# Attention and two Strassen-like MLPs on one core: order of the reciprocals, of the loads and of one product, and the place of some tiles

## What is computed

```python
scores = cap * np.tanh(scale * (q @ k.T) / cap)
attn = np.exp(scores - max);  attn = attn / (attn.sum(-1) + 1e-9);  x = attn @ v
h = x @ w_in;  g = np.maximum(0.01 * h, h);  x = g @ w_out            # 768 -> 2048 -> 768
xn = x / rms * rms_g;  g = xn @ w_gate;  silu = g / (1 + np.exp(-g))
out = (silu * (xn @ w_val)) @ w_out2                                   # 768 -> 1536 -> 768
```

## Time and profile before

| | us |
|---|---|
| three executions, median | 560.29 |
| lowest, highest | 560.08, 561.92 |
| the profiled execution: device time | 560.67 |
| its span, first to last instruction | 558.9 |
| PE busy | 553.1 (99%) |
| DVE busy | 429.7 (77%) |
| POOL busy | 323.6 (58%) |
| ACT busy | 290.0 (52%) |

### The profile page before, as it was taken

How to read it: one execution, slowest core, us unless ns; L and a number is a source line. 1 busy time by engine, 2 the same in 40 slices (tenths; PEclk the granted TensorE clock), 3 DMA queues, 4 the chain that set the end, 5 groups by cost and what they waited for, 6 DMA issues and landing times.

```text
span 558.9 us, 7933 instructions
## 1 busy us (share of the span) xinstructions
PE 553.1 (99%) x2679; PEld 466.1 (83%) x2679; DVE 429.7 (77%) x594; ACT 290.0 (52%) x503; POOL 323.6 (58%) x282
## 2 busy tenths in 40 slices
PE   8999999999999999999999999999999999999997
PEld 5545554699999999999999999999999999999896
DVE  4459988695677799932159498999999999999963
ACT  6888889326445497431155355444434446824330
POOL 1025365478666653594383576766776896634672
PEclk9999999999999999999999999999999999999999
DMA  6254442123111112213022011122211111210521
GB/s 174 70 177 149 135 133 52 37 72 110 62 56 57 57 57 66 86 38 114 1 62 90 0 58 56 58 65 86 77 56 57 57 57 57 62 52 1 154 91 67
DMA packets 30007, 41.49 MB, mean 74 GB/s; under 512 B 17040, under 2 KB 19088, under 8 KB 29968
## 3 DMA queue, kind: packets, MB, share of 16 engines
q1 hardware_dynamic: 29824, 40.99, 23.7%
q10 hardware_dynamic: 144, 0.00, 0.0%
HBM read 38.15 MB, written 2.80 MB: 73 GB/s over the span
## 4 chain that ended last, share of the span: by engine, by line
PE 90%; DVE 6%; issue 2%; DMA 1%; ACT 0%; DVEq 0%; ACTq 0%
PE ps L1763 46%; PE ps L1848 13%; PE ps L1696 9%; PE ps L1933 8%; PE ps L1835 7%; PE ps L1684 3%; PE ps L1702 2%; PE ps L1688 1%; DVE act_lo L1502 1%; DVE x_lo L1502 1%; DMA qk_raw<-in_qk 1%; DVE x_lo_f L1476 1%; DVE act_full L1482 0%; DMA sums<-x_raw 0%; DVE x_raw L1069 0%
## 5 line engine op out<-in xcount | busy, mean ns | idle before, releaser
L644 POOL TENSOR_TENSOR w_lo<-w_raw,w_hi 128x384 fp32r<-128x384 f32 x109 | 128.6, 1189 | 82.3 <-ACT w_hi L757 81.6
L644 POOL TENSOR_TENSOR w_lo<-s_sum,w_hi 128x384 fp32r<-128x384 f32 x112 | 129.6, 1172 | 78.9 <-ACT w_hi L757 78.8
L1763 PE MATMUL ps<-x_hi,w_hi 128*128 128x448 f32 x420 | 154.1, 367 | 0.0
L1763 PE MATMUL ps<-x_hi,w_lo 128*128 128x448 f32 x420 | 153.5, 365 | 0.0
L1763 PE MATMUL ps<-x_lo,w_hi 128*128 128x448 f32 x420 | 153.4, 365 | 0.0
L757 ACT ACTIVATE w_hi<-s_sum 128x384 fp32r<-128x384 f32 x112 | 57.1, 523 | 125.4 <-DVE s_sum L1132 50.1
L1763 PEld LDWEIGHTS ps<-x_hi,w_hi 128*128 128x128 f32 x420 | 78.9, 188 | 7.3 <-issue 0.7
L1763 PEld LDWEIGHTS ps<-x_hi,w_lo 128*128 128x128 f32 x420 | 78.9, 188 | 6.4
L1763 PEld LDWEIGHTS ps<-x_lo,w_hi 128*128 128x128 f32 x420 | 78.9, 188 | 6.2
L757 ACT ACTIVATE w_hi<-w_raw 128x384 fp32r<-128x384 f32 x109 | 55.0, 512 | 20.2 <-PE ps L1835 10.0
L1696 PE MATMUL ps<-probs,v_ones 128*65 128x448 f32 x144 | 56.6, 540 | 0.3 <-DVE x_raw L1069 0.2
(11 more groups left out here) (220 smaller groups left out, 1086.1 us busy)
## 6 DMA issues: line engine op xcount, KB each, us to landing
w_raw<-in_w_out SPq DMA_DIRECT2D x27, 384.0 KB, 3.5
w_raw<-in_w_in SPq DMA_DIRECT2D x16, 384.0 KB, 3.8
qk_raw<-in_qk SPq DMA_DIRECT2D x11, 480.0 KB, 4.5
w_raw<-in_w_gate SPq DMA_DIRECT2D x12, 384.0 KB, 3.0
w_raw<-in_w_val SPq DMA_DIRECT2D x12, 384.0 KB, 3.7
v_ones<-in_v SPq DMA_DIRECT2D x12, 224.0 KB, 3.2
recip_row<-recips SPq DMA_DIRECT2D x12, 224.0 KB, 3.4
out<-sq SPq DMA_DIRECT2D x6, 224.0 KB, 2.0
```

The source lines that it names most:

```text
L644: pool.tensor_tensor(w_lo[:, c], source, w_hi[:, c].bitcast(F32), ALU.subtract).then_inc(w_lo_done, 1)
L1763: last = pe.matmul(ps[:, base(s) + BANK_OF[j], 0:S], w[:, w_c], x[:, xs(j, c)], start=(j in (P1, P5, P7, P6) and c == 0 and w is w_hi and ...
```

## The change

It has seven parts. (1) In DVE's loop of the pairs, `normalise(p - 2)` stands ahead of `reciprocal(p - 1)`. (2) On SP, q and k of pair 4 are loaded ahead of the loop and those of pair p + 5 behind `store_recip(p)`. (3) On SP, panel p instead of p - 1 is loaded in turn p, and behind `load_recip_row(p)`, for p from 0 to 3. (4) The eight small tiles are laid behind G and `spare`, which moves RING, G and `spare` down by 352 bytes, to multiples of 256 bytes from the base. (5) The low part of (1, `T2`, 2) gets a place of its own, `z_spare` in `spare`; it is made before `z_sum(1, T4, 2)` and waits for it no more. (6) At the joint PE makes `P1` of unit 1 before column 2 of `P3`, `P7` and `P6` of unit 0. (7) The order of counts `pe_order` follows (6).

```diff
-    pe_order = [widx(0, j) for j in (P1, P5, P3, P7)] + [widx(1, P1), widx(0, P6)] + [widx(1, j) for j in (P5, P7, P6)]
+    pe_order = [widx(0, P1), widx(0, P5), widx(1, P1)] + [widx(0, j) for j in (P3, P7, P6)] + [widx(1, j) for j in (P5, P7, P6)]
...
+        RING = place["at"]
+        h_sums = buf("h_sums", 8 * S, F32)
+        G = place["at"]
+        g = buf("g", 2 * N1 * S, F32)
+        SPARE = place["at"]
+        spare = buf("spare", S, F32)
+
         ones = buf("ones", 2, F32)
...
         rms = buf("rms", 3 * 8, F32)
-        RING = place["at"]
-        h_sums = buf("h_sums", 8 * S, F32)
-        G = place["at"]
-        g = buf("g", 2 * N1 * S, F32)
-        spare = buf("spare", S, F32)
...
+            if (part, blk, c) == (1, T2, KH - 1):
+                return z_spare[:, :]
...
             load_qk(3)
+            load_qk(4)
+
             for p in range(PAIRS):
                 spread_sums(p)
                 if p + 2 < PAIRS:
                     load_v(p + 2)
-                if p + 4 < PAIRS:
-                    load_qk(p + 4)
-                if 0 < p < 5:
-                    load_raw(p - 1, w_in[p - 1])
                 store_recip(p)
+                if p + 5 < PAIRS:
+                    load_qk(p + 5)
                 load_recip_row(p)
+                if p < 4:
+                    load_raw(p, w_in[p])
...
+                if p > 1:
+                    normalise(p - 2)
                 if p > 0:
                     reciprocal(p - 1)
                 if p > 1:
-                    normalise(p - 2)
                     combine(p - 2)
...
-                if (part, blk) in ((0, T2), (0, B21), (1, T2)):
+                if (part, blk) in ((0, T2), (0, B21)) or (part, blk) == (1, T2) and c < KH - 1:
                     dve.wait_ge(t4_done[part], c + 1)
...
-            for c in range(KH):
+            for c in range(KH - 1):
                 z_sum(1, T4, c)
                 z_lo(1, T2, c)
+            z_lo(1, T2, KH - 1)
+            z_sum(1, T4, KH - 1)
...
-            for j in (P3, P7):
-                product(0, j, last_c)
             pe.wait_ge(x_raw_done, PAIRS)
             product(1, P1)
-            product(0, P6, last_c)
+            for j in (P3, P7, P6):
+                product(0, j, last_c)
```

More of the change, by code:

```diff
@@ L166, in build @@
         z_acc_lo = buf("z_acc_lo", S, F32R)
+        at(SPARE)
+        z_spare = buf("z_spare", S, F32R)
         at(XL)
```

## The result

The changed kernel takes 562.27 us, the median of 20 executions (560.53 to 565.87), against 560.88 us of the kernel before (20 executions, 560.08 to 563.35) beside it. The ratio is 1.0024, interval 1.0013 to 1.0035: it is slower by 1.4 us, where the prediction had it 2.7 us faster. The profiled execution of the changed kernel is one of its quick ones (560.87 us, span 559.1), so its trace shows where time went, but less of it than the median lost.

The account below looks back on a forecast made before the run. PE was taken as the bound, busy 553.1 of 558.9 us. Gains 0.32 + 0.28 + 0.08 + 0.98 + 0.46 + 0.62 = 2.74 us took the median 560.29 to 557.6 us, range 556.8 to 559.5.

Parts of the forecast that it names:

- the step that failed: Attention: the reciprocals' store and load have some 8 us, since `normalise` uses them one turn later.
- the 0.40 us: Attention: DVE's idle time for pair 3's sums, to be filled by the product by the reciprocals.
- The term of +0.32: Attention: PE's wait at the weighing of pair 6 goes, as DVE's copies come sooner; gain 0.32 us.
- sums behind the panels: Rival, attention: sums land late behind panels, q and k ahead of the reciprocals' load; 563.3 us, chance 0.05.
- The joint: Between units 0 and 1: no wait at `P7`, quick rhythm stays, second wait grows 0.04 us; net gain 0.28 us.
- The price of 0 for (1, `P7`): Joint: later split of the weights of (1, `P7`) costs 0; if that fails, the 0.28 us go back.
- The tiles: Aligned operands give 202.7 ns per matmul: 0.08 and 0.98 us in `w_out`, 0.46 at the end, 0 in attention.
- the 0.46 us at the end: Behind 518 us: 183 matmuls each gain 2.5 ns from aligned tiles, 0.46 us.
- My grid of 64: Matmuls were taken as slower where operands lie 32 bytes off the others' grid of 64; 202.7 ns if all share one.
- the first one, 559.1 us: Rival, alignment does nothing: the `w_out` pace comes from something else; gain 1.22 us, 559.1 us, chance 0.16.
- the second: Rival, slow rhythm: aligned streams stay at 206.9 ns in `w_out` and at the end; 560.5 us, chance 0.07.
- `T2`'s half: Last units, near 517 us: low part of (1, `T2`, 2) made first; gain 0.62 us, bounds 0.4 and 0.7.

Follow-up runs that it names:

- e13: Kernel before with the new order of loads and DVE's new order alone (parts 1 to 3): 564.17 us, ratio 1.0049 to the kernel before.
- e7: Kernel before with SP's new order of loads alone (parts 2 and 3): 560.81 us, ratio 1.0002 to the kernel before.
- e3: Changed kernel with DVE's old order, reciprocal(p - 1) ahead of normalise(p - 2) again: 559.41 us, ratio 0.9965 to the kernel before.
- e2: Changed kernel with SP's order of loads as before: 559.30 us, ratio 0.9964 to the kernel before.
- e11: Changed kernel with SP's loads and the joint as before, keeping tiles, T2's half and DVE's new order: 560.77 us, ratio 0.9995 to the kernel before.
- e14: Changed kernel with the loads as before and the small tiles ahead of the regions again: 560.98 us, ratio 0.9998 to the kernel before.
- e1: Kernel before with the moved tiles and T2's half alone (parts 4 and 5): 559.97 us, ratio 0.9975 to the kernel before.
- e5: Kernel before with the eight small tiles laid behind the regions, nothing else (part 4): 559.65 us, ratio 0.9970 to the kernel before.
- e6: Changed kernel with loads and DVE's order as before, keeping tiles, T2's half and the joint's new order: 559.75 us, ratio 0.9969 to the kernel before.
- e12: Kernel before with one 32-byte tile laid behind the regions, moving them down by 32 bytes: 559.47 us, ratio 0.9976 to the kernel before.
- e10: Changed kernel with q and k loaded as before and only the panels moved: 559.21 us, ratio 0.9972 to the kernel before.
- e4: Changed kernel with the old order at the joint: 560.51 us, ratio 0.9991 to the kernel before.
- a3: Changed kernel itself, run a third time on one chip with its old-joint version: 562.86 us, ratio 1.0020 to the kernel before.
- a1: Changed kernel itself, run again for the spread of its executions: 562.67 us, ratio 1.0025 to the kernel before.
- e8: Changed kernel with the eight small tiles back ahead of the regions: 565.96 us, ratio 1.0073 to the kernel before.
- e15: Changed kernel with the old order at the joint, second run, beside the changed kernel on one chip: 562.63 us, ratio 1.0032 to the kernel before.

## Why the prediction was wrong

**Attention: the step that failed.** "What is late next is the store and load of the reciprocals; `normalise` uses them one turn later, so they have some 8 us." They had that in the kernel before, where the next reciprocal doesn't stand behind `normalise`. Part 1 of the change puts it there, and the 8 us then have to hold the whole round: 1.9 us to the issue of the row's load, 5.1 us for its landing, 1.5 us of DVE (means of pairs 1 to 6 in the changed kernel). That is 8.5 us in each round, against PE's 8.05. I looked at who fills the 0.40 us and not at which loop the exchange closes. The row's load had 3.3 us in the trace of before; the text itself names q and k ahead of it, and gives that no price of its own. The term of +0.32 came out as a loss of 0.7 us in attention and 0.8 at the joint in the profiled execution, and e13 against e7 puts DVE's new order on top of the new loads at 3.4 us in the medians, 2.6 by the ratios.

Nor did the panel's move bring the 0.32. With the new loads no turn waits for a panel, but DVE waits longer for the sums (in e7 1.40 us for pair 3's, where it was 0.40), and pair 6 still waits, 0.59 us from start to start in e7 and 0.56 in e3, for 0.52 before. With the old loads and DVE's new order it is gone (0.20 in e2, e11 and e14). And in part it was a matter of one execution: in e1, e5, e6 and e12, which change neither loads nor DVE's order, it is 0.26 to 0.30. The trace of one execution was all I read.

**The rival that came near in time** was "sums behind the panels", with 0.05 and 563.3, which is 1.0 us from the median measured. That is luck. The sums did come 1.7 us later (4.17 for 2.48), but from pair 1 to pair 9 of the changed kernel DVE stood for the row of the reciprocals and never for the sums, and e10, with the panels ahead of the sums, is no slower than e2. What mattered of this rival is its half sentence "and q and k ahead of the reciprocals' load", which was given no price.

**The joint.** 0.28 us were forecast. Where pair 10 was in time, in e6 and e2, there is no rhythm of 206.8 between the two waits, and the joint took 24.50 and 24.44 us, where e1, e3 and e5 took 24.59 in the old order at the slow rhythm: 0.1 to 0.15. But the kernel before took 24.45, and e12 24.16, in the old order and at the quick rhythm, so even this is not told from the traces' spread. The price of 0 for (1, `P7`) held. What I had not seen are the 31st matmul, which waits for the take of `P5`, and with it for DVE's work on pair 10, and the first matmul of (1, `P5`): it waits, 0.39 to 0.84 us from start to start, in eight of the ten traces with the new order at the joint, all but e2 and e6.

**The tiles** were the term that held. 0.98 + 0.08 us were forecast for the `w_out` stage, 1.09 measured (111.55 for 112.64), and no gain in attention, as said (e14 against e2). The whole of it is 1.36 us in the medians of e5, forecast 1.52, but that nearness is partly luck: the interval reaches from 0.7 to 2.7 us, and e5's own trace has 1.09 less in `w_out` and 0.32 more at the end. Of the 0.46 us at the end some 0.4 came in the changed kernel (202.7 ns) and none in e1, e3, e4, e5 and a3, whose last pieces ran at 206.7; a3 is the changed kernel itself. My grid of 64 was too narrow (e12). The rival that the page's rule of 16 bytes leads to is the first one, 559.1 us, and not the second as the text has it.

**`T2`'s half** was mis-sized: 0.62 forecast, 0.25 in the traces. DVE's timeline and PE's at that place, to be held against the earlier trace rows:

```profile
517.40 0.62 DVE L1512 TENSOR_TENSOR z_spare<-act_full,x_hi 128x448 fp32r<-128x448 f32 x1
517.93 0.62 DVE L1503 TENSOR_TENSOR act_full<-act_full 128x448 f32<-128x448 f32 x1
518.47 0.62 DVE L1165 TENSOR_TENSOR a_t<-ps,p 128x448 f32<-128x448 f32 x1
```

```profile
517.54 0.47 PE L1944 MATMUL ps<-x_hi,w_hi 128*128 128x448 f32 x1 [0.17 <-DVE act_lo L1512]
...
519.23 0.44 PE L1944 MATMUL ps<-x_hi,w_hi 128*128 128x448 f32 x1 [0.20 <-DVE a_t L1165]
```

The wait moved to (1, `T2`, 1), as forecast, and `T2`, 2 follows without one. But six matmuls on, PE's next product needs the bank that the take of `P5` frees, and stands 0.37 us from start to start. I had written that this take is delayed by nothing; true, but PE comes to it sooner, and that I did not follow.

**Noise.** The result's interval is 0.1% to either side, narrower than the 0.3% that I took, but single executions of the changed kernel spread over 5.3 us. What I left out is that a rhythm of 206.7 on a whole stage (a1, +1.8 us; the rest of `w_in` at 79.76 to 79.78 instead of 78.23 in e7, e8 and e15) comes and goes from execution to execution.

## What to carry to other kernels

Before two steps of an engine change places, draw the loop that runs through them over DMAs and the next turn: its length must fit in one period of the bounding engine, and putting the step that consumes a round trip ahead of the step that feeds the next one can halve the periods it has. Price two parts of a change together where one takes the slack that the other needs: the new loads alone changed nothing here (e7), DVE's new order with the old loads nothing beside the new joint (e2 against e6), together they cost about 3 us. Try the regions that PE streams from at multiples of 256 bytes.

The version with the lowest median is the changed kernel with q and k loaded as before and only the panels moved (e10, 559.21 us, 0.28% faster than before). It can't be told from the one with all loads as before (e2, 559.30), from the one with DVE's old order (e3, 559.41), nor from the kernel before with moved tiles alone (e12, 559.47; e5, 559.65).

## What the runs showed of the chip

- The pace of 448-column matmuls that take their moving tiles from several regions by turns depends on where the regions start: 204.9, 203.7 and 202.7 ns in the `w_out` stage for RING and G at an odd multiple of 32, at a multiple of 64 but not of 128, and at a multiple of 256 bytes from the base, with the same instructions (before, e12, e5).
- A stream with all tiles on the grid has two rhythms, 202.7 and 206.7 ns, and keeps the one it is in to the next wait, over 180 matmuls in the last piece and 450 in `w_out` (a1). It is not set by the kernel's text: the changed kernel ran its last 180 matmuls in 36.72 us in its first trace and in 37.45 in a3. What sets it no run shows.
- A load issued behind large ones lands late. In e13 the row, 224 KB, issued 1.0 us after q and k of 480 KB, landed 5.83 us after its issue and 1.25 us after theirs; from pair 7 on, with no q and k left to load, the rows of the same trace took 3.2 to 3.6 us. The Trainium skill, page "DMA: Bandwidth & Descriptors", section "Queues, rings and completion order", has each engine's descriptors consumed in ring order, though a later one may finish its write first; here the order of landing is that of issue (36.94, then 38.19).
